# Pooled attention and channel mix on one core: one unit with eight products instead of two, token sums, their low parts and the next statistics moved into the last pair of the attention

## What is computed

```python
# q, k, v: (4, 8, 1152, 64); attention of pooled queries
q_pool = q.reshape(B, H, S // 2, 2, D).mean(axis=3)          # 576 queries
scores = (1 / sqrt(D)) * q_pool @ k^T
attn = exp(scores - max) / (sum + 1e-9)
o = attn @ v                                                  # (4, 8, 576, 64)
x = o.transpose(0, 2, 1, 3).reshape(4, 576, 512)
# layer norm, channel mix, residual
xn = (x - mean) / sqrt(var + 1e-6) * g_ln
out = x + relu(xn @ w_ch1) @ w_ch2                            # 512 -> 2048 -> 512
```

## Time and profile before

| | |
|---|---|
| median of 3 runs | 813.35 us (811.8 to 813.62) |
| the profiled execution | 812.01 us, its span 810.3 us |
| TensorE busy | 796.0 us, 98% of the span |
| VectorE, ScalarE, POOL busy | 643.2, 417.7, 446.1 us (79%, 52%, 55%) |
| granted TensorE clock | 1.000 (mean) |

### The profile page before, as it was taken

One profiled execution on the slowest core, in us unless ns is written; L12 is line 12 of the kernel. 1 busy time (PEld: TensorE's weight loads), 2 busy tenths in 40 slices (PEclk: granted clock), 3 DMA queues, 4 the chain that ended last, 5 costly groups with the idle time before them and its releaser, 6 DMA issues. The chain is left out here.

```text
span 810.3 us, 17080 instructions
## 1 busy us (share of the span) xinstructions
PE 796.0 (98%) x6488; PEld 665.4 (82%) x6488; DVE 643.2 (79%) x990; ACT 417.7 (52%) x941; POOL 446.1 (55%) x341
## 2 busy tenths in 40 slices
PE   8999999999999999999999999999999999999998
PEld 6777778787778777788779899989888989999897
DVE  6788888888898999888567967898877788766654
ACT  4676556675566765667723445453335444432431
POOL 3988898888898888887794212331321333122100
PEclk9999999999999999999999999999999999999999
DMA  8566443566444665311112121213321122421212
GB/s 187 133 146 142 118 90 95 140 146 145 100 95 99 146 146 129 76 62 51 32 53 63 62 86 53 63 56 105 116 66 53 53 92 66 142 79 56 62 40 78
DMA packets 39681, 75.36 MB, mean 93 GB/s; under 512 B 8880, under 2 KB 23472, under 8 KB 36016
## 3 DMA queue, kind: packets, MB, share of 16 engines
q1 hardware_dynamic: 38128, 73.88, 34.9%
q10 hardware_dynamic: 1472, 0.39, 0.3%
HBM read 69.54 MB, written 4.72 MB: 92 GB/s over the span
## 5 line engine op out<-in xcount | busy, mean ns | idle before, releaser
L579 POOL TENSOR_TENSOR acc<-acc,pT 128x576 f32<-128x576 f32 x160 | 238.4, 1490 | 23.2 <-ACT pT L911 0.4
L1261 PE MATMUL banks<-w2f,hT 128*128 128x512 f32 x864 | 214.3, 393 | 0.0
L911 ACT ACTIVATE pT<-banks 128x576 f32<-128x576 f32 x288 | 171.8, 653 | 36.8 <-PE banks L711 31.2
L1261 PEld LDWEIGHTS banks<-w2f,hT 128*128 128x128 f32 x864 | 160.3, 188 | 28.8 <-issue 0.2
L1021 DVE TENSOR_REDUCE pm<-banks 128x2 f32<-128x1024 f32 x128 | 153.2, 1221 | 37.3 <-PE banks L657 36.0
L713 PE MATMUL banks<-qT,kT 64*128 64x288 f32 x1728 | 162.1, 298 | 3.4 <-DVE pm L1021 2.3
L713 PEld LDWEIGHTS banks<-qT,kT 64*128 64x128 f32 x1728 | 133.5, 184 | 18.7 <-DVE pm L1021 7.5
L724 PE MATMUL banks<-pT,vn 128*64 128x288 f32 x1152 | 146.1, 408 | 0.0
L1339 ACT ACTIVATE hT<-mid 128x384 fp32r<-128x384 f32 x88 | 46.4, 527 | 184.1 <-DVE mid L1406 182.8
L391 POOL TENSOR_TENSOR w_sums<-w_stage 128x256 f32<-128x256 f32 x22 | 17.2, 783 | 211.1 <-DMA w_stage<-in_moe_w_ch_dram 211.1
L1406 DVE TENSOR_TENSOR mid<-banks,mid 128x384 f32<-128x384 f32 x154 | 85.5, 555 | 57.4 <-PE banks L1250 53.4
(11 more groups left out here) (120 smaller groups left out, 973.2 us busy)
## 6 DMA issues: line engine op xcount, KB each, us to landing
q_in_rows<-in_q_dram SPq DMA_DIRECT2D x56, 284.0 KB, 6.5
k_in_rows<-in_k_dram SPq DMA_DIRECT2D x56, 284.0 KB, 5.1
w_stage<-in_moe_w_ch_dram SPq DMA_DIRECT2D x24, 512.0 KB, 3.8
w_stage<-in_moe_w_ch_dram SPq DMA_DIRECT2D x48, 256.0 KB, 2.7
vn<-in_v_dram SPq DMA_DIRECT2D x16, 576.0 KB, 5.0
out_dram<-x SPq DMA_DIRECT2D x16, 256.0 KB, 3.2
q_in_rows<-in_q_dram SPq DMA_DIRECT2D x4, 256.0 KB, 3.1
k_in_rows<-in_k_dram SPq DMA_DIRECT2D x2, 288.0 KB, 4.1
```

The costliest lines, as they stand in the source:

```text
L579: nc.gpsimd.tensor_tensor(total, pT[:, h % 2, 0] if kt == 1 else total, pT[:, h % 2, kt], ALU.add).then_inc(chained, 1)
L911: nc.scalar.activation(pT[:, h % 2, kt], pair_banks("S", n)[:, :, 0:HW], ACT.Exp, scale=SCALE).then_inc(exp_done, 1)
L1261: last = nc.tensor.matmul(banks[:, k % 2 * (CT // 2) + kk], hT[:, k, a, tokens], w2f[:, (2 * u + k // 2) % 4, b], start=p == 0 and k < 2 a ...
```

## The change

`PLAIN` goes from 2 to 1: unit 1 is a seven-product unit now, with 42 matmuls of products instead of 48, seven weight forms instead of four, and all token forms needed one unit earlier. For that the token sums T1 and T2 are made by POOL ahead of the last pair's totals, T3 and T4 by VectorE at the end of its last pair. VectorE makes the high and low parts of B12, B22, T1 and T2 and the low parts of B11 and B21 before `add_end` of the last pair's first half. The statistics of part 1, moments and epsilon are made at the end of VectorE's last pair. T3's high part stands ahead of ScalarE's unit 0.

```diff
-    PLAIN = 2
+    PLAIN = 1
@@ attention_gpsimd
             for j in range(PAIRS):
+                if j == PAIRS - 1:
+                    sum_tokens(nc.gpsimd, pool, 0, T1)
+                    sum_tokens(nc.gpsimd, pool, 0, T2)
                 add_up(2 * j)
                 add_up(2 * j + 1)
@@ attention_vector
-                if j == PAIRS - 2:
-                    tokens_lo(nc.vector, dve, 0, B11)
-                    tokens_lo(nc.vector, dve, 0, B21)
@@ last_pair_vector
             j = PAIRS - 1
+            for i in (B12, B22):
+                tokens_hi(dve, nc.vector.tensor_copy, 0, i)
+            for i in (B12, B22, B11, B21):
+                tokens_lo(nc.vector, dve, 0, i)
             for at in range(4):
                 weights_lo(0, at)
+            for i in (T1, T2):
+                tokens_hi(dve, nc.vector.tensor_copy, 0, i)
+                tokens_lo(nc.vector, dve, 0, i)
             add_end(dve, 2 * j)
-            for i in (B12, B22):
-                tokens_hi(dve, nc.vector.tensor_copy, 0, i)
-            for i in (B12, B22):
-                tokens_lo(nc.vector, dve, 0, i)
             take_end(j + 1)
             scale_outputs(j - 2)
             add_end(dve, 2 * j + 1)
             take_end(j + 2)
             scale_outputs(j - 1)
+            sum_tokens(nc.vector, dve, 0, T3)
+            sum_tokens(nc.vector, dve, 0, T4)
+            dve.wait_ge(x_written, 3 * PAIRS // 4)
+            for kk in range(CT):
+                statistics(1, kk)
+            moments_of(1)
+            variance_eps(1)
+            tokens_lo(nc.vector, dve, 0, T3)
@@ mix_gpsimd
-            sum_tokens(nc.gpsimd, pool, 0, T1)
-            sum_tokens(nc.gpsimd, pool, 0, T2)
             pool.wait_ge(scored, KT * HALVES)
             sum_weights(nc.gpsimd, pool, PLAIN)
-            sum_tokens(nc.gpsimd, pool, 0, T3)
-            sum_tokens(nc.gpsimd, pool, 0, T4)
-            for u in range(1, UNITS):
+            sum_weights(nc.gpsimd, pool, PLAIN + 1)
+            inverse_deviation(1)
+            for u in range(PLAIN, UNITS):
...
-                if u % FP == 2 and u // FP + 1 < PARTS:
+                if u % FP == 2 and 1 < u // FP + 1 < PARTS:
                     inverse_deviation(u // FP + 1)
@@ mix_scalar
+            tokens_hi(act, nc.scalar.copy, 0, T3)
             for u in range(PLAIN):
...
-                for i in ((T2, T1), (T3,))[u]:
-                    tokens_hi(act, nc.scalar.copy, 0, i)
@@ mix_vector (next_tokens, next_tokens_within: units 1 and 2)
-                if p == 1:
+                if p == 1 and n > 1:
...
-                if p == 2:
+                if p == 2 and n > 1:
...
-                for i in ((T2, T1), (T3,))[u]:
-                    tokens_lo(nc.vector, dve, 0, i)
-                next_tokens(u)
```

## The result

The changed kernel takes 817.5 us (median of 5 runs, 817.12 to 818.59), the kernel before 813.32 beside it (5 runs); the ratio is 1.0059, 95% interval [1.0047, 1.007]. By the ratio the change made the kernel slower by 4.8 us (3.8 to 5.7); 3.9 us and 817.3 were predicted. The profiled execution of after took 818.59 us (span 816.9), of before 812.01. The traces run alike up to the border of the phases, where after's is 0.38 us later than before's (the last `xg_b` of part 0 at 389.60 against 389.22); times of after are compared with this in mind.

What follows compares the result with a forecast made beforehand. TensorE was taken to bound the second phase, leaning on POOL's totals and VectorE's queue at the phase border. A first down product 5.7 us late minus 1.84 gave +3.9: 817.3 against the median, range 813.0 to 820.5.

Steps and rivals of the forecast that it cites:

- The likeliest case: Backlog of VectorE and POOL at the border of the phases: kernel slower by 2.6 to 6 us; chance 0.62.
- Step 1: Before `add_end(30)`: VectorE gets about one instruction in per POOL instruction; POOL's last add of half 30 at 412.1, +4.1 us.
- Step 2: Half 31 and row sums: POOL's totals ready at 425.3, product 2 of unit 0 at 427.6 after `h_lo` 1, +4.1 us.
- Step 3: Sums of weights for unit 1: S2 at 428.0 holds `h_lo` 2 until 430.1; product 3 at 430.2, +4.5 us.
- Step 4: First down product waits for `x` until 436.4, +5.7 us; the 1.05 us of saved matmuls lies inside that wait.
- Step 5: Unit 2, first seven-product unit of before: moving statistics, moments and epsilon removes its wait, -1.84 us; T4's low part stays.
- Sum: Whole kernel: 5.7 - 1.84 = +3.9 us, 817.3 against the median; bounds at the first down product alone +2.6 to +4.8.
- Faster: VectorE and POOL fit the added work into idle times; `add_end(30)` done by 407.96, -2.9 us, 810.5; chance 0.09.
- no change: Half the backlog shows: first down product 0.5 to 3.4 us late, net -1.3 to +1.6, about 813.5; chance 0.17.
- Clock: TensorE's standstill of 4 us brings 1.2 GHz; 24 matmuls of products 2 and 3 take 8.6 us, 821; chance 0.08.
- The stall doesn't go: T4's low part and the late middle stall unit 1 instead; the 1.84 us isn't gained, 819.2; chance 0.04.

Runs made afterwards that it cites:

- Experiment 4: Changed kernel with `add_end(30)` directly behind the four low parts of B, T1's and T2's casts and low parts behind the last scaling; 821.13 us, ratio 1.0109.
- experiment 5: Changed kernel with 16 transposes of the identity into an unread bank on TensorE ahead of the last row sums; 818.29 us, ratio 1.0066.
- experiment 2: Changed kernel with `PLAIN` back at 2, the rest of the change kept; 816.57 us, ratio 1.0052.
- Experiment 1: Kernel before with only part 1's statistics, moments and epsilon moved to the end of VectorE's last pair; 810.74 us against 812.21, ratio 0.9979.
- experiment 3: Changed kernel with statistics, moments, epsilon and POOL's inverse of the deviation back where the kernel before has them; 817.13 us, ratio 1.0062.
- experiment 9: Relaid one-plain-unit kernel: T1's, T2's sums in VectorE's idle time, T3's, T4's on POOL between sums of weights, statistics back in units 1 and 2; 812.01 us, ratio 0.9997.
- experiment 10: Experiment 9 with VectorE taking `h_lo`, scaling and w2 part before weight forms, POOL both sums of weights before T3's and T4's; 812.6 us, ratio 0.9997.
- Experiment 8: Kernel before with only POOL's T1 and T2 token sums moved ahead of the last pair's totals; 815.83 us against 811.98, ratio 1.0038.
- experiment 7: Changed kernel laid out anew: `add_end(30)` behind the weights, T1's, T2's casts on ScalarE, T3's, T4's sums on POOL, weight forms later; 816.2 us, ratio 1.0047.

## Why the prediction was right, point by point

The likeliest case came about, by its own chain, with the steps late by 0.9 to 1.7 us. Predicted against measured, the latter less the 0.38 us of the later start:

- **Step 1**, POOL's last add of half 30: 412.1, measured 413.14. The mechanism is the one given: no hole in POOL, VectorE one instruction to each of POOL's, then 3.69 us of idle POOL. Experiment 4 bears it out: with `add_end(30)` taken first POOL's idle time goes, and the row sums come 2.9 us earlier. The size was low by 1.0 us: beside VectorE's wide low parts the token sums took 2.56 and 2.37 us, not 1.98, and those parts 2.34 each, not 2.1. Beside the 256-column parts five totals took 8.17 us, 1.63 each, so POOL lost almost nothing there, and VectorE, whose part of 0.36 us took 1.58, paid nearly everything. The Trainium skill (SBUF - State Buffer, Who interferes with whom) has the two exclude each other for the whole instruction; the trace agrees in kind, and shows that the cost isn't shared evenly.
- **Step 2**, row sums: 425.3, measured 426.7; product 2: 427.6, measured 428.95. The row sums have step 1's 1.0 us and some 0.3 more of longer totals. Product 2 was to wait for `h_lo` 1 until 427.6; it waited for the row sums instead, which took 2.29 us instead of 1.27 at a lower clock.
- **Step 3**, product 3 held by S2: S2 was there at 429.67 (428.0 predicted), `h_lo` 2 at 431.2 (430.1). With product 2 itself late and slow, product 3 followed it without a wait of its own; experiment 5 shows the wait for `h_lo` 2, 0.83 us, once product 2 runs at full clock.
- **Step 4**, first down product: 436.4, measured 437.27; the wait for `x` behind only six matmuls, 1.62 us, is the one given, and experiment 2 shows that the saved 1.05 us lies in it. From `h_lo` 2 to the last scaling VectorE took 5.9 us (431.60 to 437.50), predicted 6.2, so the step itself held and what it inherited was 1.1 us late.
- **Step 5**, -1.84: unit 2 took 15.59 against 17.47, so -1.88. The size held, the cause was told too narrowly. I put the wait down to the statistics and left T4's low part where it was, though with `PLAIN` 1 it goes to unit 1. Experiment 1 takes away the statistics alone, experiments 3, 9 and 10 take away T4's low part (and T3's) and leave the statistics, and unit 2 takes 15.59 to 15.62 us in all four. So the wait takes both together, and the change holds two cures for it.
- **Sum**: +3.9 predicted, +4.7 measured in the trace at the end of unit 2. The upper bound that step 4 alone gives was added wrongly: 436.7 - 430.67 - 1.84 is +4.2, not +4.8, and the measured +4.7 lies above it, since steps 1 to 3 were late. That 817.3 and 817.5 are so near is in part luck: between the medians lie 4.2 us, by the ratio it is 4.8. Unit 10 of the profiled execution has another 1.4 us (a wait of 1.35 against 0.33 us for a late `mid`). That execution was after's slowest, so the medians, 4.2 us apart, need not hold it; whether it belongs to the change stays open.

What the prediction didn't see is how little of the change is needed for a loss. It counted the work on VectorE ahead of `add_end(30)`, 14 instructions, as the load that makes it late. Experiment 8 adds none to it and loses 0.38%, some 1.7 of its 3.8 us by a fallen clock: POOL's hole of 3.49 us had been the time in which VectorE's weights ran at their own speed, and without it the last E and O of TensorE wait for the scaling. In after TensorE is 2.0 us late in the same place, a part of the 4.4 us by which its row sums are late that the prediction's steps don't name. And in experiment 4 what wasn't paid ahead of `add_end(30)` was paid behind it.

**The rivals.** *Faster* and *no change* needed POOL's last add of half 30 at 408; it came at 413.52. *Clock*: the granted clock did fall. A window of after (us, each engine's busy time with PE, PEld, DVE, ACT, POOL in this order, granted clock, DMA share, GB/s):

```profile
424.00:430.00 6.00, 3.58 (x30) 3.06 (x30) 4.71 (x14) 0.00 (x0) 5.84 (x5) 0.75 0.13 46
```

It was 0.75 from 424 to 430 us and 0.96 in the next window, so a part of the time at 1.2 GHz, behind a wait of 2.42 us. I gave this 0.08. The fall happened, the price didn't: the 24 matmuls took 4.99 us and not 8.6, and in experiment 5's trace, where the clock holds, `down(0, 0)` comes no earlier, since VectorE's `x` ends last either way. *The stall doesn't go*: it went.

## What to carry to other kernels

An engine's idle time has a second use: it is when its neighbour runs at full speed. Before a hole is filled, look at what the other engine does in it; here two POOL instructions of 2 us put into a hole of 3.5 cost VectorE 6.78 - 1.42 = 5.4 us and the kernel 0.38%, the clock that fell behind TensorE's waits included. A wait that several pieces of work cause together goes away with any one of them: move the one that has idle time to go to (the statistics, -0.21%), alone, and measure before the rest follows. And where a saved matmul has a waiting instruction behind it, it is worth nothing until that wait is gone.

## What the runs showed of the hardware that was not expected

- VectorE beside POOL. A low part of 256 columns takes 0.36 us alone, 1.58 beside POOL's adds of 576 columns, and 2.06 beside a sum of 768. A cast of 768 columns takes 0.4 to 0.5 us alone and 1.76 beside POOL. In these rows VectorE's instruction takes about as long as POOL's, whatever its own length. Not every instruction of VectorE is held so: the six statistics took 0.61 us each beside POOL's totals in after (3.65 from 422.56) and in experiment 1 (3.66), where those totals, five in 7.98 us, were no slower than before's 7.96.
- The clock after short waits. In experiments 3, 7 and 8 two waits, of 0.66 to 0.81 and 1.02 to 1.03 us, stand ahead of the last value product, and its 36 matmuls take 6.27 or 6.28 us instead of 4.59, with a granted clock of 0.86 from 412 to 418 us and 0.85 from 418 to 424 in experiment 8. After has nearly the same two waits, 0.65 and 1.03 us, experiment 2 has 0.70 and 1.03, experiment 5 has 0.66 and 1.02 just as experiment 3, and all three kept their clock there. What tells them apart was not found.
- In experiment 4 the clock fell to 0.66 (424 to 430 us) and 0.50 (430 to 436), in the latter window 1.2 GHz throughout; once TensorE was kept busy the kernel was 0.27% shorter. In after the same remedy gave nothing by the trace: there VectorE's `x` ended last.
